# The second token group's seven taps summed by VectorE, and the first group's last sums taken in halves

## The chip, the cores and the metric

The kernel runs on one core of a Trainium2 chip. The metric is the device time of one execution in microseconds (us). Engines are named as in the profile: PE is TensorE, PEld its weight loads, DVE is VectorE, ACT is ScalarE, POOL is GpSimd and SP is SyncE, which here only issues DMAs.

## What is computed

A softmax-weighted causal convolution of 7 taps runs over the tokens, and a feed-forward layer follows it. Cut to what matters (B, S, D = 4, 4096, 192; H = 8 heads of 24 channels, K = 7 taps, d_ff = 2048):

```python
w = exp(weight_gen - max(weight_gen)); w = w / (sum(w) + 1e-9)      # per token and head, 7 taps
x_pad = concatenate([zeros(B, 6, D), x], axis=1)
conv[b, s, h, :] = sum over k of w[b, s, h, k] * x_pad[b, s + k, h, :]   # 24 channels a head
h = conv.reshape(16384, 192) @ w_in                                   # 192 -> 2048
g = where(h >= 1, h, where(h <= -1, 0, (h + 1)**2 / 4))
out = g @ w_out                                                       # 2048 -> 192
```

All values are fp32. The matmuls run in a reduced format (fp32r), so that each operand is split into a high part and a low part (what the high part leaves over), and products of high with high, low with high and high with low are added.

## The kernel before

**Layout.** The 16384 tokens lie in 32 lanes, and the 192 channels in 4 quads of 48, which gives 128 partitions. A group is 512 tokens (16 steps of each lane); there are 32 groups, worked in 16 pairs: `b` is 0 or 1 inside pair `pair`. Of a quad's 48 channels 32 are the main part and 16 the rest part. After the convolution a group is transposed by DVE, in blocks of 32 by 32, into `main_turn` and `rest_turn`; `xt_high` and `xt_low` are the high and low part of the turned main part, `xt_rest` holds both parts of the rest.

**The feed-forward loop.** For each group the 2048 hidden units are 16 tiles, n = 0 to 15. Tile n takes five matmuls into one of four PSUM banks (`slot`; line 815), by high and low weights `in_main_high`, `in_main_low`, `in_rest_high`, `in_rest_low`. Then ACT takes half_relu (L557), ACT squares it (L563), DVE clips it in place (L675, the gate), ACT copies the high part out (L568, gate_high) and DVE subtracts it (L681, gate_low). PE multiplies the gates of tile n - 4 with `out_parts`, the high and low part of w_out, in eight matmuls (L841), right after the hidden products of tile n (`LAG = 4`). PE may write tile n's slot only once the gate_low of tile n - 4 is done. Each engine works a queue written out by hand; what an engine does besides the tiles is put between two tiles by tables such as `HIGHS_AFTER`.

**The convolution.** In the loop POOL makes the convolution of the next group: seven products of `x_in` with a tap weight (L381) and six additions (L410, L418), all 128x768. The head of the program is different: group 0's convolution is made by DVE (taps 0 to 4) and POOL (taps 5 and 6), and PE adds the pieces with an identity matrix as stationary operand into PSUM (L851 main part, L854 rest part). Group 1 is convolved by POOL while PE works the 16 tiles of group 0.

**The weights.** High and low parts of w_in and w_out are made during the head and group 0, in pieces: ACT makes the high parts (`in_high`, `out_high`), and the low parts are subtractions. `in_low` pieces 0 to 3 (for tiles 0 to 7) are made by POOL in the head, pieces 4 to 7 by DVE after its gates of tiles 3, 4, 8 and 9 (L485). The four `out_low` pieces (L491) are POOL's. Piece c of `out_low` is needed by PE's outputs of tile 4c:

```python
wait(pe, gate_low_done, pair, 2 * NT, NT * b + n + 1)
if b == 0 and is_first(pair) and n % CT == 0:
    pe.wait_ge(out_low_done, n // CT + 1)
```

**Around the second group.** `rest_high` (ACT, L576) copies the rest part's high half, `rest_low` (POOL, L469) subtracts, DVE turns it (L712); the main part is turned (L702), copied (`main_high`, L581) and subtracted (`main_low`, L476).

## Time and profile before

| what | value |
| --- | --- |
| median of 3 runs | 1200.57 us (1200.52 to 1203.15) |
| the profiled execution's own time | 1203.05 us |
| span of the profiled execution | 1201.2 us |
| PE busy | 1191.7 us (99%) |
| DVE, ACT, POOL busy | 803.8 (67%), 899.9 (75%), 782.5 us (65%) |
| chain that ended last, by engine | PE 97%, DVE 1%, ACT 1% |

The span is the time from the first to the last instruction; the execution's own time has 1.85 us more, which lie outside it. The chain that ended last is followed back from the last instruction, at each step to what released it, so its shares say which engine sets the end. Of the three runs two lie at 1200.5 and one at 1203.15; the profiled one lies beside the third.

### The profile page before, as it was taken

The page shows a single profiled execution, that of the slowest core. Times are in us where ns is not written, and L with a number is a line of the kernel's source. Part 1 is how long each engine was busy: PE and PEld are TensorE (multiplying, and loading weights), DVE is VectorE, ACT ScalarE, POOL GpSimd, SP SyncE. Part 2 cuts the span into 40 slices and gives each one's busy share as a digit, 9 for nine tenths or more (in the row PEclk, how much of TensorE's full clock was granted, in tenths as well). Part 3 has the DMA queues.
Part 4 walks back from the last instruction along what each step waited for, and adds up shares of the span by engine and source line. Part 5 has one row for each costly group of instructions (what it writes and reads, how often), then busy time and mean ns, then how long its engine had stood idle before and what let it go on. Part 6 is the DMA issues. An engine that isn't in the chain of part 4 may idle for free.

```text
span 1201.2 us, 21341 instructions
## 1 busy us (share of the span) xinstructions
PE 1191.7 (99%) x6716; PEld 1071.9 (89%) x6716; DVE 803.8 (67%) x1331; ACT 899.9 (75%) x1775; POOL 782.5 (65%) x547
## 2 busy tenths in 40 slices
PE   8999999999999999999999999999999999999998
PEld 6889999898899999999989999899999998989888
DVE  6876666666666666666666666666666666666665
ACT  5877777777777777777777777777777777777775
POOL 7888577655677555776556776557765567765500
PEclk9999999999999999999999999999999999999999
DMA  8202122210222201222102222012221022220000
GB/s 170 40 13 57 21 44 44 44 40 4 44 44 44 44 22 21 44 44 44 35 8 44 44 44 44 22 21 44 44 44 35 8 44 44 44 44 22 1 36 14
DMA packets 172247, 45.33 MB, mean 38 GB/s; under 512 B 161220, under 2 KB 163652, under 8 KB 172228
## 3 DMA queue, kind: packets, MB, share of 16 engines
q1 hardware_dynamic: 167284, 44.29, 17.4%
q10 hardware_dynamic: 4944, 0.80, 0.5%
q8 instruction: 10, 0.16, 0.1%
q14 instruction: 9, 0.07, 0.0%
HBM read 24.62 MB, written 12.58 MB: 31 GB/s over the span
## 4 chain that ended last, share of the span: by engine, by line
PE 97%; DVE 1%; ACT 1%; POOL 0%; DMA 0%; issue 0%; ACTq 0%; DVEq 0%; POOLq 0%
PE slot L815 49%; PE acc L841 48%; DVE in_main_low L485 0%; DMA gen_in<-in_weight_gen 0%; PE slot L851 0%; POOL conv L528 0%; ACT gate_high L568 0%; ACT square L563 0%; POOL conv L381 0%; POOL out_cross L381 0%; DVE slot L675 0%; DVE gate_low L681 0%; ACT half_relu L557 0%; DVE out_sb L719 0%; PE acc L854 0%
## 5 line engine op out<-in xcount | busy, mean ns | idle before, releaser
L841 PE MATMUL acc<-out_parts,gate_high 128*128 128x384 f32 x2048 | 613.1, 355 | 0.0
L681 DVE TENSOR_TENSOR gate_low<-slot,gate_high 128x512 fp32r<-128x512 f32 x512 | 353.9, 691 | 384.1 <-ACT gate_high L568 384.1
L841 PE MATMUL acc<-out_parts,gate_low 128*128 128x192 f32 x2048 | 513.3, 251 | 0.0
L557 ACT ACTIVATE half_relu<-slot 128x512 f32<-128x512 f32 x512 | 308.1, 602 | 255.9 <-PE slot L815 248.8
L841 PEld LDWEIGHTS acc<-out_parts,gate_high 128*128 128x128 f32 x2048 | 384.8, 188 | 30.0 <-DVE out_sb L719 8.4
L841 PEld LDWEIGHTS acc<-out_parts,gate_low 128*128 128x128 f32 x2048 | 390.1, 190 | 18.4
L675 DVE SCALAR_TENSOR_TENSOR slot<-slot,square 128x512 f32<-128x512 f32 x512 | 353.2, 690 | 1.2 <-ACT square L563 1.2
L568 ACT ACTIVATE gate_high<-slot 128x512 fp32r<-128x512 f32 x512 | 304.0, 594 | 29.2 <-DVE slot L675 28.2
L563 ACT ACTIVATE square<-half_relu 128x512 f32<-128x512 f32 x512 | 324.4, 634 | 0.0
L381 POOL TENSOR_TENSOR tap<-x_in,tap_w 128x768 f32<-128x768 f32 x186 | 286.6, 1548 | 0.0
L410 POOL TENSOR_TENSOR conv<-conv,tap 128x768 f32<-128x768 f32 x124 | 229.5, 1851 | 0.0
L815 PE MATMUL slot<-xt_high,in_main_high 128*128 128x512 f32 x512 | 211.8, 414 | 3.2 <-DVE gate_low L681 3.1
L815 PE MATMUL slot<-xt_low,in_main_high 128*128 128x512 f32 x512 | 202.3, 395 | 0.1
L815 PE MATMUL slot<-xt_rest,in_rest_high 128*128 128x512 f32 x512 | 201.2, 393 | 0.0
L815 PE MATMUL slot<-xt_high,in_main_low 128*128 128x512 f32 x512 | 201.1, 393 | 0.0
L815 PE MATMUL slot<-xt_rest,in_rest_low 128*128 128x512 f32 x512 | 199.2, 389 | 0.0
L469 POOL TENSOR_TENSOR rest_parts<-conv,rest_parts 128x256 fp32r<-128x256 f32 x31 | 23.3, 751 | 174.6 <-ACT rest_parts L576 96.9
L815 PEld LDWEIGHTS slot<-xt_rest,in_rest_low 128*128 128x128 f32 x512 | 96.3, 188 | 23.2
L815 PEld LDWEIGHTS slot<-xt_rest,in_rest_high 128*128 128x128 f32 x512 | 96.0, 188 | 22.1
L815 PEld LDWEIGHTS slot<-xt_low,in_main_high 128*128 128x128 f32 x512 | 96.2, 188 | 21.6 <-DVE xt_low L476 0.5
L815 PEld LDWEIGHTS slot<-xt_high,in_main_high 128*128 128x128 f32 x512 | 96.3, 188 | 4.2 <-DVE gate_low L681 3.7
L815 PEld LDWEIGHTS slot<-xt_high,in_main_low 128*128 128x128 f32 x512 | 97.8, 191 | 0.1
(66 smaller groups left out, 532.1 us busy)
## 6 DMA issues: line engine op xcount, KB each, us to landing
x_in<-in_x SPq DMA_DIRECT2D x122, 132.0 KB, 3.0
out<-out_sb SPq DMA_DIRECT2D x31, 384.0 KB, 2.9
xt_rest<-rest_turn SPq DMA_DIRECT2D x30, 256.0 KB, 2.3
gen_in<-in_weight_gen SPq DMA_DIRECT2D x122, 28.0 KB, 2.2
out_raw<-in_moe_w_out SPq DMA_DIRECT2D x4, 384.0 KB, 5.1
in_main<-in_moe_w_in SPq DMA_DIRECT2D x8, 64.0 KB, 3.8
in_main<-in_moe_w_in SPq DMA_DIRECT2D x4, 128.0 KB, 4.4
in_rest<-in_moe_w_in SPq DMA_DIRECT2D x4, 128.0 KB, 4.4
```

What stands on the lines that cost most here:

```text
L381: return ops.tensor_tensor((dst if isinstance(dst, bass.AP) else dst[:]).rearrange("p t (h c) -> p t h c", h=HQ), x_in[b][:, k:k + STEP, : ...
L410: nc.gpsimd.tensor_tensor(to[:], conv[b][:], tap[k % 3][:], ALU.add).then_inc(conv_step, 1)
L469: return ops.tensor_tensor(rest_half(1), conv[b][:, :, MAIN:CH], rest_half(0).bitcast(F32), ALU.subtract)
L557: nc.scalar.activation(half_relu[n % 2][:], tile_slot(n)[:], ACT.Relu, scale=0.5, bias=0.5).then_inc(relu_done, 1)
L563: nc.scalar.activation(square[n % 2][:], half_relu[n % 2][:], ACT.Square).then_inc(square_done, 1)
L568: nc.scalar.activation(gate_high[GATE_AT[n]][:], tile_slot(n)[:], ACT.Copy).then_inc(gate_high_done, 1)
L675: nc.vector.scalar_tensor_tensor(h[:], h[:], 1.0, square[n % 2][:], ALU.max, ALU.min).then_inc(gate_done, 1)
L681: nc.vector.tensor_tensor(gate_low[GATE_AT[n]][:], tile_slot(n)[:], gate_high[GATE_AT[n]][:].bitcast(F32), ALU.subtract).then_inc(gate_low ...
L815: ins = nc.tensor.matmul(tile_slot(n)[:], w[:, units], xt[b][:], start=(j == 0), stop=(j == len(products) - 1))
L841: ins = nc.tensor.matmul(dst, stationary, moving, start=(n == 0 and j == 0), stop=(n == NT - 1 and j == 1))
```

## The change

Three things are changed. All lie in the head and in pair 0; the loop over the other pairs is the same code.

1. **Second group.** POOL makes only the seven products, into `second_taps`, a buffer with eight planes of 128x768. DVE adds them with six reductions over the tap axis (`second_sum`), whose innermost read step is one plane (768 elements). Three of them add planes 0 to 3 into plane 7 (the rest channels, then the main channels of steps 0 to 7, then of steps 8 to 15), after the gates of tiles 5, 6 and 7; three add planes 4 to 7 into `conv1`, after the gates of tiles 9, 10 and 11. Each makes 256 sums of 4 elements. `rest_high` comes after tile 10 on ACT, `rest_low` after it on POOL, the rest part is turned after tile 11, and its copy to `xt_rest` goes by DMA in place of ACT.
2. **Low parts.** `in_low` 4 to 7 move from DVE to POOL. `out_low` 2 moves from the middle of POOL's convolution to behind `rest_low`.
3. **First group.** Taps 5 and 6, whose sum POOL now adds in two halves (steps 0 to 7 and 8 to 15), are added by DVE and no longer by PE; the last sums, their transposes, `xt_high` and `xt_low` go in halves through two PSUM banks. PE's order in tiles 0 and 1 has the rest products ahead of the xt_low product. The second group's weight_gen is loaded after in_rest's second piece on ACT's DMA queue, and its exponent is taken after `xt_rest`.

```diff
-IN_LOWS_AFTER = {3: 4, 4: 5, 8: 6, 9: 7}
-HIGHS_AFTER = {1: ("out", 1), 2: ("in", 4), 3: ("in", 5), 5: ("out", 2), 7: ("in", 6), 8: ("in", 7),
+HIGHS_AFTER = {1: ("out", 1), 2: ("in", 4), 3: ("in", 5), 5: ("in", 6), 6: ("in", 7), 7: ("out", 2),
                9: ("out", 3)}
-OUT_LOWS_AFTER_TAP = {1: 1, 3: 2}
+EARLY_TAPS = 4
+SECOND_SUMS_AFTER = {5: (0, 0), 6: (0, 1), 7: (0, 2), 9: (1, 0), 10: (1, 1), 11: (1, 2)}
-FIRST_MAIN_AFTER, FIRST_REST_AFTER = (12, 9), (12, 12)
+FIRST_MAIN_AFTER, FIRST_REST_AFTER = (12, 9), (11, 12)
+SECOND_REST_HIGH_AFTER = 10
 SOFTMAX_AFTER = {2: ("max",), 7: ("sum", "inverse")}
-FIRST_SOFTMAX_AFTER = ({5: ("max",), 11: ("sum", "inverse")}, {2: ("max",), 10: ("sum", "inverse")})
-EXP_AFTER, FIRST_EXP_AFTER = 7, (11, 10)
-PAD_AFTER_TAP, SHIFT_AFTER_TAP = 2, 4
+FIRST_SOFTMAX_AFTER = ({8: ("max",), 13: ("sum", "inverse")}, {2: ("max",), 10: ("sum", "inverse")})
+EXP_AFTER, FIRST_EXP_AFTER = 7, (12, 10)
...
+        HALF = STEP // 2
+        first_main = [slot[i][:, 0:HALF * MAIN].rearrange("p (t c) -> p t c", c=MAIN) for i in (3, 1)]
+        first_turned = [t[:, 0:GT // 2].rearrange("p (i j r) -> p i j r", i=TOK, r=LANES) for t in (slot[2], acc[0])]
         first_rest = acc[TOK - 1][:, 0:STEP * REST].rearrange("p (t c) -> p t c", c=REST)
...
-                    if has_next(pair, b) and not (b == 0 and is_first(pair)):
+                    if has_next(pair, b):
...
+        def convolve_second(pool):
+            def taps(first, last):
+                for k in range(first, last):
+                    tap_product(nc.gpsimd, 1, k, second_taps[:, k]).then_inc(second_tap_made, 1)
+            pool.wait_ge(x_loaded[1], 16 * QUADS)
+            pool.wait_ge(taps_ready, 2)
+            taps(0, EARLY_TAPS)
+            out_low(pool, nc.gpsimd, 1).then_inc(out_low_done, 1)
+            in_low(pool, nc.gpsimd, 4).then_inc(in_low_done, 1)
+            in_low(pool, nc.gpsimd, 5).then_inc(in_low_done, 1)
+            pool.wait_ge(first_conv_done, 1)
+            nc.gpsimd.memset(x_in[0][:, 0:PAD, :], 0.0).then_inc(x_padded, 1)
+            taps(EARLY_TAPS, K)
+            in_low(pool, nc.gpsimd, 6).then_inc(in_low_done, 1)
+            in_low(pool, nc.gpsimd, 7).then_inc(in_low_done, 1)
...
                 if is_second(pair, b):
-                    out_low(pool, nc.gpsimd, W_CHUNKS - 1).then_inc(out_low_done, 1)
+                    out_low(pool, nc.gpsimd, 2).then_inc(out_low_done, 1)
+                    shift(pool, nc.gpsimd, *after(pair, b))
+                    out_low(pool, nc.gpsimd, 3).then_inc(out_low_done, 1)
...
-                nc.gpsimd.tensor_tensor(conv[1][:], conv[1][:], partial, ALU.add).then_inc(late_tap_step, 1)
+                for i in range(2):
+                    nc.gpsimd.tensor_tensor(steps_half(conv[1], i), steps_half(conv[1], i), steps_half(partial, i),
+                                            ALU.add).then_inc(late_tap_step, 1)
...
-                wait_conv(act, pair, b)
+                if is_second(pair, b):
+                    act.wait_ge(second_rest_summed, 1)
+                else:
+                    wait_conv(act, pair, b)
...
+            def first_main_high(i):
+                act.wait_ge(first_main_turned if i == 0 else main_turned, 1)
+                nc.scalar.activation(first_columns(xt_high[0], i), first_turned[i], ACT.Copy
+                                     ).then_inc(first_xt_high_done if i == 0 else xt_high_done, 1)
...
             for q in range(QUADS):
+                load_rest(act, 1, q)
+            for q in range(QUADS):
                 load_gen(act, 0, 1, q)
-            for q in range(QUADS):
-                load_rest(act, 1, q)
...
-            exponent(0, 1)
+            first_main_high(0)
             rest_high(0, 0)
-            main_high(0, 0)
+            first_main_high(1)
             out_high(0)
             act.wait_ge(rest_turned, 1)
             nc.scalar.activation(xt_rest[0][:], rest_turn[:], ACT.Copy).then_inc(first_xt_rest_done, 1)
+            exponent(0, 1)
...
-                        if n == main_after(pair, b) and has_next(pair, b):
+                        if n == rest_high_after(pair, b) and has_next(pair, b):
                             rest_high(*after(pair, b))
                         if n == main_after(pair, b) + 1 and has_next(pair, b):
                             main_high(*after(pair, b))
-                        if b == 0 and is_first(pair) and n == rest_after(pair, b) + 1:
-                            act.wait_ge(rest_turned, 2)
-                            nc.scalar.activation(xt_rest[1][:], rest_turn[:], ACT.Copy).then_inc(xt_rest_copied, 16)
...
+            def second_sum(late, piece):
+                steps, chans = ((slice(0, STEP), slice(MAIN, CH)), (slice(0, HALF), slice(0, MAIN)),
+                                (slice(HALF, STEP), slice(0, MAIN)))[piece]
+                taps = slice(EARLY_TAPS, K + 1) if late else slice(0, EARLY_TAPS)
+                to = conv[1][:] if late else second_taps[:, K]
+                dve.wait_ge(second_tap_made, K if late else EARLY_TAPS)
+                if late:
+                    dve.wait_ge(second_early_summed, piece + 1)
+                if late and piece == 2:
+                    dve.wait_ge(second_rest_summed, 1)
+                    dve.wait_ge(second_main_summed, 1)
+                done = (second_rest_summed, second_main_summed, conv_done)[piece] if late else second_early_summed
+                nc.vector.tensor_reduce(to[:, steps, chans],
+                                        second_taps[:, taps, steps, chans].rearrange("p k t c -> p t c k"),
+                                        AX.X, ALU.add).then_inc(done, 1)
...
+                for i in range(2):
+                    nc.vector.tensor_tensor(first_fourth[i], first_fourth[i], steps_half(tap[2], i), ALU.add
                                             ).then_inc(first_conv_step, 1)
-                tap_product(nc.vector, 0, 4, tap[2], first_taps_w).then_inc(first_conv_step, 1)
-                dve.wait_ge(first_conv_step, 4 + HQ)
-                dve.wait_ge(first_tap_summed, 1)
-                for h in range(HQ):
-                    nc.vector.tensor_tensor(head(conv[0], h), first_fourth[h], head(tap[2], h), ALU.add
+                    dve.wait_ge(first_conv_step, 7 + 2 * i)
+                    dve.wait_ge(late_tap_step, LATE + i + 1)
+                    nc.vector.tensor_tensor(steps_half(conv[0], i), first_fourth[i], steps_half(conv[1], i), ALU.add
                                             ).then_inc(first_conv_step, 1)
...
+            first_turn_main(0)
             softmax(0, 1, "max")
-            shift(dve, nc.vector, 0, 1)
-            turn_main(0, 0)
+            first_turn_main(1)
             dve.wait_ge(rest_high_done, 1)
             nc.vector.tensor_tensor(rest_half(1), first_rest, rest_half(0).bitcast(F32), ALU.subtract
                                     ).then_inc(first_rest_low_done, 1)
             turn_rest(0, 0)
-            dve.wait_ge(xt_high_done, 1)
-            main_low(nc.vector, 0, 0).then_inc(first_xt_low_done, 1)
+            shift(dve, nc.vector, 0, 1)
+            for i in range(2):
+                dve.wait_ge(first_xt_high_done if i == 0 else xt_high_done, 1)
+                nc.vector.tensor_tensor(first_columns(xt_low[0], i), first_turned[i],
+                                        first_columns(xt_high[0], i).bitcast(F32), ALU.subtract
+                                        ).then_inc(first_xt_low_done, 1)
...
-            sum_tap(conv[0], first_conv_step, 1, first=True)
-            sum_tap(tap[0], first_conv_step, 2)
-            sum_tap(tap[1], first_conv_step, 3)
-            sum_tap(conv[1], late_tap_step, LATE + 1)
-            sum_tap(conv[0], first_conv_step, 4 + 2 * HQ, last=True)
+            sum_tap(conv[0], 1, first=True)
+            sum_tap(tap[0], 2)
+            sum_tap(tap[1], 3)
+            pe.wait_ge(first_conv_step, 8)
+            sum_main(conv[0], 0, last=True)
+            pe.wait_ge(first_conv_step, 10)
+            sum_rest(conv[0], last=True)
+            sum_main(conv[0], 1, last=True)
             warm(WARM_PRODUCTS[1])
             for n in range(2):
-                hidden_products(0, 0, n, 0, 2)
+                hidden_products(0, 0, n, (0, 1), opens=True, closes=False)
             for n in range(2):
-                hidden_products(0, 0, n, 2, 3)
+                hidden_products(0, 0, n, (3, 4, 2), opens=False, closes=True)
```

On POOL, from the end of the head to the end of its work for the second group, the instructions stood so before (L381 products, L410 and L418 additions, L491 out_low pieces 1, 2 and 3, L469 `rest_low`):

```order
L410 TENSOR_TENSOR conv<-conv,tap 128x768 [waits conv_step]
L491 TENSOR_TENSOR out_parts<-out_raw,out_parts 128x4x192 [waits out_high_done]
L381 TENSOR_TENSOR tap<-x_in,tap_w 128x768
L410 TENSOR_TENSOR conv<-conv,tap 128x768 [waits conv_step]
L452 TENSOR_TENSOR gen_shift<-gen_in,gen_max 128x224 [waits exp_done,max_done]
L381 TENSOR_TENSOR tap<-x_in,tap_w 128x768
L410 TENSOR_TENSOR tap<-conv,tap 128x768 [waits conv_step]
L418 TENSOR_TENSOR conv<-tap 128x768 [waits conv_step]
L469 TENSOR_TENSOR rest_parts<-conv,rest_parts 128x256 [waits rest_high_done]
L491 TENSOR_TENSOR out_parts<-out_raw,out_parts 128x4x192 [waits out_high_done]
L476 TENSOR_TENSOR xt_low<-main_turn,xt_high 128x512 [waits xt_high_done]
```

Here the first L491 is `out_low` 2, which waits for nothing but its high part. In the changed kernel (L394 products, L510 in_low pieces 4 to 7, L516 out_low pieces, L495 `rest_low`):

```order
L394 TENSOR_TENSOR second_taps<-x_in,tap_w 128x768 x3
L516 TENSOR_TENSOR out_parts<-out_raw,out_parts 128x4x192 [waits out_high_done]
L510 TENSOR_TENSOR in_main_low<-in_main,in_main_high 128x512 [waits in_high_done]
L510 TENSOR_TENSOR in_rest_low<-in_rest,in_rest_high 128x512 [waits in_high_done]
L439 MEMSET x_in 128x288 [waits first_conv_done]
L394 TENSOR_TENSOR second_taps<-x_in,tap_w 128x768 x3
L510 TENSOR_TENSOR in_main_low<-in_main,in_main_high 128x512 [waits in_high_done]
L510 TENSOR_TENSOR in_rest_low<-in_rest,in_rest_high 128x512 [waits in_high_done]
L495 TENSOR_TENSOR rest_parts<-conv,rest_parts 128x256 [waits rest_high_done]
L516 TENSOR_TENSOR out_parts<-out_raw,out_parts 128x4x192 [waits out_high_done]
L475 TENSOR_TENSOR gen_shift<-gen_in,gen_max 128x224 [waits exp_done,max_done]
L516 TENSOR_TENSOR out_parts<-out_raw,out_parts 128x4x192 [waits out_high_done]
```

`out_low` 2, the L516 behind L495, now stands behind an instruction that waits for `rest_high_done`.

On DVE, between the gates (L675) of tiles 3 to 5, before:

```order
L675 SCALAR_TENSOR_TENSOR slot<-slot,square 128x512 [waits square_done]
L485 TENSOR_TENSOR in_main_low<-in_main,in_main_high 128x512 [waits in_high_done]
L681 TENSOR_TENSOR gate_low<-slot,gate_high 128x512 [waits gate_high_done]
L675 SCALAR_TENSOR_TENSOR slot<-slot,square 128x512 [waits square_done]
L485 TENSOR_TENSOR in_rest_low<-in_rest,in_rest_high 128x512 [waits in_high_done]
L681 TENSOR_TENSOR gate_low<-slot,gate_high 128x512 [waits gate_high_done]
```

and in the changed kernel from the gate (L713) of tile 5 to that of tile 8 (L719 is gate_low, L756 the new reductions):

```order
L713 SCALAR_TENSOR_TENSOR slot<-slot,square 128x512 [waits square_done]
L756 TENSOR_REDUCE second_taps<-second_taps 128x16x16 [waits second_tap_made]
L719 TENSOR_TENSOR gate_low<-slot,gate_high 128x512 [waits gate_high_done]
L713 SCALAR_TENSOR_TENSOR slot<-slot,square 128x512 [waits square_done]
L756 TENSOR_REDUCE second_taps<-second_taps 128x8x32 [waits second_tap_made]
L719 TENSOR_TENSOR gate_low<-slot,gate_high 128x512 [waits gate_high_done]
L713 SCALAR_TENSOR_TENSOR slot<-slot,square 128x512 [waits square_done]
L756 TENSOR_REDUCE second_taps<-second_taps 128x8x32 [waits second_tap_made]
L719 TENSOR_TENSOR gate_low<-slot,gate_high 128x512 [waits gate_high_done]
L713 SCALAR_TENSOR_TENSOR slot<-slot,square 128x512 [waits square_done]
L699 TENSOR_REDUCE gen_max<-gen_in 128x32 [waits shift_done,gen_loaded0]
```

The two L485 between the gates are gone, and three reductions have come in two tiles later.

## Rows read from the trace of the kernel before

**Rows 1.** The page: busy time by engine, and the chain by engine.

```profile
PE 1191.7 (99%) x6716; PEld 1071.9 (89%) x6716; DVE 803.8 (67%) x1331; ACT 899.9 (75%) x1775; POOL 782.5 (65%) x547
PE 97%; DVE 1%; ACT 1%; POOL 0%; DMA 0%; issue 0%; ACTq 0%; DVEq 0%; POOLq 0%
```

**Rows 2.** Waits of PE: who for whom, us in total, times, longest.

```profile
PE slot L815 <- DVE gate_low L681: 3.1, 2, 2.6
```

**Rows 3.** PE's timeline: start, us busy, and in brackets idle before.

```profile
21.86 0.50 PE L815 MATMUL slot<-xt_high,in_main_high 128*128 128x512 f32 x1 [0.46 <-DVE gate_low L681]
...
31.61 0.50 PE L815 MATMUL slot<-xt_high,in_main_high 128*128 128x512 f32 x1 [2.61 <-DVE gate_low L681]
...
53.86 0.41 PE L815 MATMUL slot<-xt_high,in_main_high 128*128 128x512 f32 x1
...
56.15 0.41 PE L815 MATMUL slot<-xt_high,in_main_high 128*128 128x512 f32 x1
```

**Rows 4.** DVE's timeline, group 0: the gates of tiles 3, 7 and 8.

```profile
25.96 0.69 DVE L675 SCALAR_TENSOR_TENSOR slot<-slot,square 128x512 f32<-128x512 f32 x1
26.56 4.39 DVE L485 TENSOR_TENSOR in_main_low<-in_main,in_main_high 128x512 fp32r<-128x512 f32 x1
...
37.62 0.69 DVE L675 SCALAR_TENSOR_TENSOR slot<-slot,square 128x512 f32<-128x512 f32 x1
39.02 0.69 DVE L681 TENSOR_TENSOR gate_low<-slot,gate_high 128x512 fp32r<-128x512 f32 x1 [0.72 <-ACT gate_high L568]
39.63 0.69 DVE L675 SCALAR_TENSOR_TENSOR slot<-slot,square 128x512 f32<-128x512 f32 x1
```

**Rows 5.** POOL's timeline, group 0.

```profile
28.60 1.79 POOL L410 TENSOR_TENSOR conv<-conv,tap 128x768 f32<-128x768 f32 x1
30.35 0.33 POOL L413 MEMSET x_in<- 128x288 f32 x1
...
34.55 1.85 POOL L491 TENSOR_TENSOR out_parts<-out_raw,out_parts 128x768 fp32r<-128x768 f32 x1
...
49.29 0.74 POOL L469 TENSOR_TENSOR rest_parts<-conv,rest_parts 128x256 fp32r<-128x256 f32 x1 [3.01 <-ACT rest_parts L576]
```

**Rows 6.** Windows: busy PE, PEld, DVE, ACT, POOL; granted clock; DMA share, GB/s.

```profile
32.00:36.00 4.00, 4.00 (x15) 3.63 (x14) 3.36 (x7) 3.81 (x7) 4.00 (x3) 0.57 0.47 82
```

**Rows 7.** The head's timeline: DVE, PE and ACT.

```profile
11.38 1.02 DVE L739 TENSOR_TENSOR conv<-acc,tap 128x384 f32<-128x384 f32 x2
...
14.76 0.73 DVE L702 STREAM_TRANSPOSE slot<-slot 128x512 f32<-128x512 f32 x1 [1.63 <-PE slot L851]
...
16.18 0.50 PE L815 MATMUL slot<-xt_high,in_main_high 128*128 128x512 f32 x1
...
16.84 0.63 ACT L622 ACTIVATE xt_rest<-rest_turn 128x512 fp32r<-128x512 f32 x1
...
17.43 0.50 PE L815 MATMUL slot<-xt_low,in_main_high 128*128 128x512 f32 x1
```

**Rows 8.** Groups of instructions by form: busy us, mean ns, idle before.

```profile
L665 DVE TENSOR_REDUCE gen_sum<-gen_exp 128x32 f32<-128x256 f32 x31 | 12.7, 410 | 0.5 <-ACT gen_exp L552 0.5
...
L702 DVE STREAM_TRANSPOSE main_turn<-conv 128x512 f32<-128x512 f32 x31 | 34.5, 1111 | 0.0
```

**Rows 9.** ACT's timeline, group 0.

```profile
39.91 0.61 ACT L557 ACTIVATE half_relu<-slot 128x512 f32<-128x512 f32 x1
40.39 0.62 ACT L568 ACTIVATE gate_high<-slot 128x512 fp32r<-128x512 f32 x1
40.86 0.66 ACT L563 ACTIVATE square<-half_relu 128x512 f32<-128x512 f32 x1
41.38 0.87 ACT L612 ACTIVATE out_parts<-out_raw 128x768 fp32r<-128x768 f32 x1
42.12 0.63 ACT L557 ACTIVATE half_relu<-slot 128x512 f32<-128x512 f32 x1
...
48.78 0.43 ACT L576 ACTIVATE rest_parts<-conv 128x256 fp32r<-128x256 f32 x1
```

119 lines of the change are left out of this document (66 added, 53 removed).

## Prediction

> **What bounds the kernel now.** I read the page first: PE is busy 99% of the span and makes 97% of the chain that ended last [rows 1]. So only two things can move the end: what PE does, which the change leaves alone, and when PE stands still or runs slow. The waits of PE come next: the longest is 2.6 us, for a gate_low [rows 2], and PE's timeline places it ahead of tile 7 of the first group, 31.61 us, 2.61 us idle [rows 3]. Then the other engines there. DVE's timeline: an `in_main_low` that began at 26.56 took 4.39 us, and the gate_low that PE wanted stood behind it [rows 4]. POOL's timeline: an addition that reads SBUF ended at 30.39, a memset began at 30.35, and DVE's subtraction ended at 30.95, 0.6 us later [rows 5]. So DVE waited for POOL with a two-input operation from SBUF, and not for its data. After the stall the windows show a granted clock of 0.57 over 32 to 36 us [rows 6], between the levels of 1.2 and 2.4 GHz: 4.00 x (1 - 0.57) = 1.72 us of PE's work is lost.
>
> From tile 4's start at 21.86 to the second group's first tile at 53.86 are 12 tiles [rows 3]. A tile at full pace is 2.29 us (53.86 to 56.15), so they would take 27.44. They took 32.00: 4.56 us are lost, of which 2.61 is the stall, 1.72 the clock, and 0.23 the restart.
>
> **The change, part by part. In_low on POOL.** DVE loses its four two-input SBUF subtractions, and with them the 4.39. All that is left of two-input work in this stretch reads PSUM with one input. This gives back the 2.61 of the stall, and the 1.95 behind it if no new stall follows. On POOL, two 128x512 subtractions take the place of two 128x768 additions ahead of the memset, so both end before the 30.35 of [rows 5], and tile 8, which needs them, starts at 30.7 (below). Then come three products and two subtractions, none longer than the 1.85 of an `out_low`: at most 9.3, to 39.6, for tile 12 at 39.86. I cost the move at nothing.
>
> **The head.** In before, PE added POOL's partial sum and then DVE's last one, and the main part was turned at 14.76 after 1.63 us of waiting; the two additions on DVE took 1.02 [rows 7]. Now DVE makes four such halves (2 x 1.02, from 11.38 to 13.43), and PE has 0.44 us of rest and a half main part left behind them, so the second main half is ready at about 14.55, 0.2 earlier. Its transpose and its copy are half as long (about 0.45 for the 0.73), so the first product comes near 15.6 for 16.18. But tile 0 also needs the rest part: high half, subtraction, transpose and the 0.63 copy, which ended at 17.47 and now ends about 0.35 earlier, at 17.1. The rest products then start there, where before PE went on at 17.43 with `xt_low` [rows 7]. Halves, warm-up and loads taken together: a gain of 0.3 us, with bounds of 0 and 0.6 (the first product's own gain).
>
> **The reductions.** Each reads 4 x 256 = 1024 elements with a step of one plane. The trace has no such read. Lower bound: the reduction of 256 elements took 0.410 us [rows 8] and a gate of 512 took 0.69 [rows 4], 1.09 ns for each element more; 768 more make 1.25 us. Upper bound: the transposes that write with a step took 1.111 us [rows 8] where the first, with runs, took 0.73 [rows 7], 0.74 ns more an element; on 1024 elements that is 0.76, so 2.01 us. I take 1.25, since it is the same operation.
>
> A rule of the Trainium skill speaks for the upper bound. Its page "Vector Engine (DVE) Microarchitecture Reference", section 5.2, measures about 1.73 ns a column where one source hops by 4 KiB at every element, against 1.05 for contiguous reads; by it a reduction would take about 1.85 us (an estimate from the page). The same section tells of a one-source operation alternating between two regions at full rate, which is why it does not settle the matter. No row here shows either.
>
> DVE's pace in this stretch is set by a ring: gate, gate_high, gate. The gates of tiles 7 and 8 are 2.01 us apart [rows 4], with 0.72 idle. A reduction of 1.25 fills the idle time: gate_low 0.61, gate 0.60, reduction 1.18 from start to start make 2.39, 0.38 more than without, and 0.10 above PE's 2.29. Gate 3 came at 25.96, 4.1 us after PE began tile 4, and PE needs its gate_low only for tile 7, 6.9 us after tile 4's start. So PE does not wait for gates here, but DVE does not catch up either.
>
> **The new wait.** `out_low` 2, which PE needs for the outputs of tile 8 (right after the hidden products of tile 12), stood at 34.55 [rows 5], 10 us early. Now it is behind `rest_low`, which waits for `rest_high`, which stands on ACT after tile 10. In steps, with the head's 0.3 off:
> - PE: tile 4 at 21.56; tile 12 at 21.56 + 8 x 2.287 = 39.86; it wants outputs 8 behind its five products, a little over half a tile, at 39.86 + 1.17 = 41.03.
> - DVE: gate 3 at 25.96 - 0.3 = 25.66 [rows 4]; gates 4 and 5 at +2.0 each, 29.66; gates 6, 7, 8 at +2.39 each, 36.83.
> - ACT: gate_high 8 at 36.83 + 0.74 = 37.57; then by the start-to-start times of [rows 9]: square 9 +0.48, `out_high` 3 +0.52, half_relu 10 +0.74, gate_high 9 +0.48, square 10 +0.47, `rest_high` +0.52: 40.78. It takes 0.43 [rows 9]: 41.21.
> - POOL: `rest_low` at 41.26, `out_low` 2 from 41.96 (0.70 on, a little under its 0.74) for 1.85 [rows 5]: 43.81. PE goes on at 43.86.
>
> PE stands 43.86 - 41.03 = 2.83 us. That is a little more than the stall that goes, so the granted clock should fall behind it as it did before: 1.95 us again with the restart.
>
> **Sum.** Stall of before -2.61, its clock and restart -1.95, head -0.3, new wait +2.83, its clock and restart +1.95: -0.08 us. Against the profiled execution's 1203.05 us this is 1203.0. That execution stands 0.2% above the median of 1200.57, beside the slowest of the three. Perhaps in the other two DVE got its turn one boundary of POOL's earlier (at 28.60 for 30.35, 1.75 us less, and with a wait of PE under 1 us perhaps no clock loss, 3.5 in all at most): they differ by 2.6. In the changed kernel this chance is gone, as no DVE operation waits for POOL's port. So I expect 1203.0 and not the same distance below the median. After tile 12 the second group's inputs are on time: the transposes of tiles 11 and 12 and `main_low` end over 1 us before PE's first product that reads them, since PE itself is late by 2.8.
>
> **Rivals.**
> - *The wait comes, the clock stays up* (0.14). The gap is a little shorter or the engine's activity around it is other than at 29 to 31 us. The sum loses 1.7: 1201.3.
> - *The strided reads are slow* (0.26, the other side). Each reduction takes 2.01; a tile with one lasts 0.61 + 0.60 + 1.94 = 3.15 on DVE. Gate 8 comes 3 x 0.76 = 2.28 later, and `rest_high` waits for the fourth reduction, about 0.6 more: PE loses 2.9 more, part of it ahead of tiles 10 and 11 on gate_low: 1203.0 + 2.9 = 1205.9. It decides from about 1.6 us a reduction. For it speak the transposes; against it, that reductions of before ran at one element a cycle. The page's rule above is this case; its 1.85 would give about 1205.3, by the same steps.
> - *No new wait* (0.12). ACT and DVE are further ahead at tile 10 than I reckon, and `out_low` 2 comes by 41.03. Then both stalls are gone: 1203.0 - 2.83 - 1.95 = 1198.2. Against it speaks gate 3's distance of 4.1 us from tile 4's start, which is of the same work in both kernels.
> - *The distance of the two kinds of runs of before has nothing to do with the stall* (0.1). Then the changed kernel's usual run lies 0.1 below the median: 1200.5.
> - *My forecast*: 0.38, its own range 1202.0 to 1204.0, by the head's bounds and 0.7 us of error in the chain.
>
> **How the numbers follow.** The range is to leave out 2 in 10: about half of the slow-reduction case above, and the better half of the no-wait case below: 1199.0 to 1206.0. About what a measurement can tell from no change here is 0.3%, 3.6 us: faster is below 1197.0, which needs no new wait and a head gain over 1 us (0.05); slower is above 1204.2, the slow-reduction case and the edge of mine (0.29); the rest is the same (0.66).
>
> **What would show it.** No L510 on DVE and no wait of PE ahead of tile 7; a wait of PE of 2.8 us near 41 us at L905, released by POOL's L516; the granted clock down for some 3 us behind it; L756 at 1.2 us; the first hidden product near 15.6 and half_relu of tile 0 near 18.1. The prediction is wrong if L756 takes over 1.6 us, if L516's third run ends before 41 us, or if PE waits for the second group's `xt_high`.

## The result, and the profile after

| kernel | median | runs | range | granted clock |
| --- | --- | --- | --- | --- |
| before | 1200.83 us | 7 | 1200.52 to 1203.23 | 0.998 in the profiled one |
| changed | 1206.17 us | 7 | 1205.54 to 1207.22 | 0.996 to 0.999 |

The changed kernel is slower: ratio 1.0039, with a 95% interval of 1.0027 to 1.0050. Its profiled execution took 1207.13 us with a span of 1205.3, 4.1 us more than before's 1201.2. The seven runs of each kernel lie in two groups, those of before at 1200.5 to 1200.8 and at 1203.1 to 1203.2, those of the changed kernel at 1205.5 to 1206.2 and at 1207.1 to 1207.2, and both profiles are of the upper group.

The page of the changed kernel, to be held against [rows 1]: busy time by engine, then the chain that ended last.

```profile
PE 1191.7 (99%) x6720; PEld 1073.1 (89%) x6720; DVE 807.8 (67%) x1337; ACT 898.9 (75%) x1775; POOL 774.9 (64%) x546
...
PE 96%; POOL 2%; issue 1%; DMA 1%; DVE 0%; ACTq 0%; ACT 0%; DVEq 0%; POOLq 0%
```

PE is busy for the same 1191.7 us, so in sum the 4.1 us are time in which PE stands still. What is new in the chain is POOL with 2%, and issue and DMA with 1% each. The waits of PE, against [rows 2]:

```profile
PE acc L905 <- POOL out_parts L516: 3.9, 1, 3.9
PE slot L879 <- DVE gate_low L719: 1.6, 3, 0.6
```

The 2.6 us for a gate_low are gone, and 3.9 us for `out_low` have come, with three shorter waits for gate_low. PE's timeline places them; against [rows 3]:

```profile
16.72 0.47 PE L879 MATMUL slot<-xt_high,in_main_high 128*128 128x512 f32 x1 [0.68 <-issue]
...
22.39 0.51 PE L879 MATMUL slot<-xt_high,in_main_high 128*128 128x512 f32 x1 [0.48 <-DVE gate_low L719]
...
36.93 0.50 PE L879 MATMUL slot<-xt_high,in_main_high 128*128 128x512 f32 x1 [0.57 <-DVE gate_low L719]
...
40.06 0.50 PE L879 MATMUL slot<-xt_high,in_main_high 128*128 128x512 f32 x1 [0.59 <-DVE gate_low L719]
...
42.44 0.41 PE L879 MATMUL slot<-xt_high,in_main_high 128*128 128x512 f32 x1
...
47.66 0.66 PE L905 MATMUL acc<-out_parts,gate_high 128*128 128x384 f32 x1 [3.88 <-POOL out_parts L516]
...
58.08 0.41 PE L879 MATMUL slot<-xt_high,in_main_high 128*128 128x512 f32 x1
```

These are tile 0's first product, tile 4, tiles 10, 11 and 12, the outputs of tile 8, and the second group's first tile. Tile 4 starts 0.53 us later than before (22.39 for 21.86). From there to the second group are 12 tiles of 2.287 us, 27.44 in all; they took 35.69, so 8.25 are lost where before lost 4.56. The two differences, 0.53 and 3.69, make 4.22, which is the span's 4.1.

DVE's timeline where the reductions stand (L756), and later the fourth of them:

```profile
30.46 0.69 DVE L713 SCALAR_TENSOR_TENSOR slot<-slot,square 128x512 f32<-128x512 f32 x1
31.06 2.06 DVE L756 TENSOR_REDUCE second_taps<-second_taps 128x256 f32<-128x1024 f32 x1
33.01 0.70 DVE L719 TENSOR_TENSOR gate_low<-slot,gate_high 128x512 fp32r<-128x512 f32 x1
33.60 0.71 DVE L713 SCALAR_TENSOR_TENSOR slot<-slot,square 128x512 f32<-128x512 f32 x1
...
42.49 1.97 DVE L756 TENSOR_REDUCE conv<-second_taps 128x256 f32<-128x1024 f32 x1
```

A reduction takes 2.06 us, and the gates before and after it (L713) are 3.14 us apart, where PE's tile takes 2.29. DVE falls behind by 0.85 us a tile. POOL's work does not make the reductions slow: the fourth takes 1.97 us while POOL stands idle (next rows). POOL's timeline behind `in_low`:

```profile
35.95 1.28 POOL L510 TENSOR_TENSOR in_rest_low<-in_rest,in_rest_high 128x512 fp32r<-128x512 f32 x1
45.00 0.73 POOL L495 TENSOR_TENSOR rest_parts<-conv,rest_parts 128x256 fp32r<-128x256 f32 x1 [7.78 <-ACT rest_parts L611]
45.69 1.82 POOL L516 TENSOR_TENSOR out_parts<-out_raw,out_parts 128x768 fp32r<-128x768 f32 x1
```

POOL stands idle for 7.78 us with `out_low` 2 (the L516 at 45.69) behind an instruction that waits for the rest part, and the rest part waits for the fourth reduction. The window from the end of PE's long wait on has, after its length, busy PE, PEld, DVE, ACT and POOL, the granted clock, and DMA share and GB/s:

```profile
46.00:52.00 6.00, 4.34 (x13) 3.96 (x14) 6.00 (x6) 2.69 (x6) 3.84 (x3) 0.50 0.01 3
```

The clock is at the lower of its two levels, 1.2 GHz, for the whole stretch. In the head, DVE's timeline against [rows 7]:

```profile
7.22 0.95 DVE L394 TENSOR_TENSOR conv<-x_in,acc 128x768 f32<-128x768 f32 x1 [0.43 <-DMA x_in<-in_x]
...
13.88 0.46 DVE L734 STREAM_TRANSPOSE slot<-slot 128x256 f32<-128x256 f32 x1
15.45 0.39 DVE L699 TENSOR_REDUCE acc<-gen_in 128x32 f32<-128x224 f32 x1 [1.11 <-DMA gen_in<-in_weight_gen]
15.75 0.45 DVE L734 STREAM_TRANSPOSE acc<-slot 128x256 f32<-128x256 f32 x1
```

The first row is DVE's first tap product. Between the two half transposes of group 0 stands the maximum of the second group's weight_gen (L699). It waited 1.11 us for its DMA, with the second half's transpose behind it.

### The profile page after: what moved, and what is told of

It is laid out like the page before. It is cut to its first block, busy times and chain, and to the rows that moved or that the text cites. A ratio compares the mean times of both kernels' runs of the same rounds, so it can differ in the third digit from the quotient of the medians.

```text
span 1205.3 us, 21360 instructions
## 1 busy us (share of the span) xinstructions
PE 1191.7 (99%) x6720; PEld 1073.1 (89%) x6720; DVE 807.8 (67%) x1337; ACT 898.9 (75%) x1775; POOL 774.9 (64%) x546
## 4 chain that ended last, share of the span: by engine, by line
PE 96%; POOL 2%; issue 1%; DMA 1%; DVE 0%; ACTq 0%; ACT 0%; DVEq 0%; POOLq 0%
PE slot L879 49%; PE acc L905 47%; POOL second_taps L394 1%; DMA gen_in<-in_weight_gen 1%; POOL out_parts L516 0%; POOL in_main_low L510 0%; POOL in_rest_low L510 0%; ACTq L297 0%; ACTq L270 0%; DVE out_sb L774 0%; DVE gen_shift L475 0%; POOL rest_parts L495 0%; DVE xt_low L820 0%; DVE gen_sum L703 0%; DVE tap_w L484 0%
## 5 line engine op out<-in xcount | busy, mean ns | idle before, releaser
L905 PE MATMUL acc<-out_parts,gate_high 128*128 128x384 f32 x2048 | 613.6, 356 | 3.9 <-POOL out_parts L516 3.9
L719 DVE TENSOR_TENSOR gate_low<-slot,gate_high 128x512 fp32r<-128x512 f32 x512 | 353.6, 691 | 384.8 <-ACT gate_high L600 384.8
L905 PE MATMUL acc<-out_parts,gate_low 128*128 128x192 f32 x2048 | 513.5, 251 | 0.0
L905 PEld LDWEIGHTS acc<-out_parts,gate_high 128*128 128x128 f32 x2048 | 385.1, 188 | 34.1 <-DVE out_sb L774 8.4
L905 PEld LDWEIGHTS acc<-out_parts,gate_low 128*128 128x128 f32 x2048 | 390.4, 191 | 18.4
L713 DVE SCALAR_TENSOR_TENSOR slot<-slot,square 128x512 f32<-128x512 f32 x512 | 353.0, 689 | 0.8 <-ACT square L595 0.8
L394 POOL TENSOR_TENSOR tap<-x_in,tap_w 128x768 f32<-128x768 f32 x180 | 277.5, 1549 | 0.0
L422 POOL TENSOR_TENSOR conv<-conv,tap 128x768 f32<-128x768 f32 x120 | 222.3, 1853 | 0.0
L495 POOL TENSOR_TENSOR rest_parts<-conv,rest_parts 128x256 fp32r<-128x256 f32 x31 | 23.1, 745 | 180.8 <-ACT rest_parts L611 97.2
```

The costliest lines, as they stand in the source:

```text
L394: return ops.tensor_tensor((dst if isinstance(dst, bass.AP) else dst[:]).rearrange("p t (h c) -> p t h c", h=HQ), x_in[b][:, k:k + STEP, : ...
L422: nc.gpsimd.tensor_tensor(to[:], conv[b][:], tap[k % 3][:], ALU.add).then_inc(conv_step, 1)
L495: return ops.tensor_tensor(rest_half(1), conv[b][:, :, MAIN:CH], rest_half(0).bitcast(F32), ALU.subtract)
L713: nc.vector.scalar_tensor_tensor(h[:], h[:], 1.0, square[n % 2][:], ALU.max, ALU.min).then_inc(gate_done, 1)
L719: nc.vector.tensor_tensor(gate_low[GATE_AT[n]][:], tile_slot(n)[:], gate_high[GATE_AT[n]][:].bitcast(F32), ALU.subtract).then_inc(gate_low ...
L905: ins = nc.tensor.matmul(dst, stationary, moving, start=(n == 0 and j == 0), stop=(n == NT - 1 and j == 1))
```

## The experiments

The first four ran on one chip, the last four on another, each beside runs of the kernel before (medians 1201.02 of 23 and 1200.71 of 24). All ratios are to before. The changed kernel was not measured again beside them, and its median of 1206.17 is the uppermost of the lower group of its runs, so differences to it below are good to about half a us.

### `out_low` 2 ahead of `rest_low`

The changed kernel with `out_low` 2 put back ahead of the wait:

```diff
             in_low(pool, nc.gpsimd, 7).then_inc(in_low_done, 1)
+            out_low(pool, nc.gpsimd, 2).then_inc(out_low_done, 1)
...
                 if is_second(pair, b):
-                    out_low(pool, nc.gpsimd, 2).then_inc(out_low_done, 1)
                     shift(pool, nc.gpsimd, *after(pair, b))
```

> The changed kernel with out_low piece 2 back ahead of rest_low on GpSimd, right after in_low 7. Theory 1 (the wait of 3.9 us sits on that piece's place): the wait at the outputs of tile 8 and the clock loss behind it go; but the second group's xt_high and xt_low stay as late as they are (ACT 53.8 us, GpSimd 54.5 to 55.8 us), so PE stands again ahead of tile 13 to 15 on gate_low and at the second group's first tile, which begins near 55 us for 58.1: 2 to 3 us faster than the changed kernel, about 1203.5. Rival (the wait is only the visible end of DVE's backlog): PE stands just as long in other places and the time does not move by more than 1 us, 1205.5 to 1206.5. Second rival (the whole loss goes): 3.9 plus the clock's 2.4, about 1200.

1204.66 us (7 runs, 1204.53 to 1205.13), ratio 1.0027, interval 1.0015 to 1.0038. The wait at L905 is gone and the clock is 1.00 from 40 to 54 us, but PE's timeline now has this:

```profile
47.78 0.50 PE L879 MATMUL slot<-xt_high,in_main_high 128*128 128x512 f32 x1 [0.61 <-DVE gate_low L719]
51.81 0.50 PE L879 MATMUL slot<-xt_high,in_main_high 128*128 128x512 f32 x1 [1.50 <-DVE gate_low L719]
```

PE waits for gate_low six times, 4.0 us in all. So the wait for `out_low` covered a second one: DVE, late by six reductions of 2 us, does not keep up either. Taking the 3.88 us wait away alone brings 1.5 us. The place of the waits is as expected (tiles 13 to 15), the time is not: the gain lies between the 2 to 3 us of the expectation and the rival's 1.

### The reductions made contiguous

The changed kernel with `second_taps` laid out with the taps innermost, so that a reduction reads four neighbouring elements for each sum, and POOL's products write with a step of eight elements:

```diff
-        second_taps = sb("second_taps", [P, K + 1, STEP, CH])
+        second_taps = sb("second_taps", [P, STEP, CH, K + 1])
...
-                    tap_product(nc.gpsimd, 1, k, second_taps[:, k]).then_inc(second_tap_made, 1)
+                    tap_product(nc.gpsimd, 1, k, second_taps[:, :, :, k]).then_inc(second_tap_made, 1)
...
-                                        second_taps[:, taps, steps, chans].rearrange("p k t c -> p t c k"),
+                                        second_taps[:, steps, chans, taps],
```

> The changed kernel with the tap axis innermost in second_taps, so that DVE's reductions read 4 neighbouring elements and GpSimd's products write with a step of 32 bytes. Theory 1 (the read's step costs 0.8 us a reduction): reductions 1.2 to 1.3 us for 2.0, the gate_low waits ahead of tiles 10 and 11 go, the wait at out_low 2 shrinks from 3.9 to about 2.8, total about 3 us faster: 1203. Rival (a sum of 4 in 1024 elements takes 2 us however it is read): reductions stay at 2.0 us and the time at 1206. Open: what the stepped writes cost GpSimd; if its products take 2.3 for 1.5 us, the four late planes come 5 us later, at 42 us, and the gain shrinks.

1202.66 us (11 runs, 1200.72 to 1204.47), ratio 1.0009, interval 1.0000 to 1.0018. The groups by form (busy us, mean ns, idle before):

```profile
L394 POOL TENSOR_TENSOR second_taps<-x_in,tap_w 128x768 f32<-128x768 f32 x7 | 11.4, 1781 | 0.0
L756 DVE TENSOR_REDUCE second_taps<-second_taps 128x256 f32<-128x1024 f32 x3 | 3.6, 1210 | 0.0
```

The same groups in the changed kernel:

```profile
L394 POOL TENSOR_TENSOR second_taps<-x_in,tap_w 128x768 f32<-128x768 f32 x7 | 10.6, 1543 | 0.3 <-DVE tap_w L484 0.3
L756 DVE TENSOR_REDUCE second_taps<-second_taps 128x256 f32<-128x1024 f32 x3 | 6.2, 2065 | 0.0
```

The reduction falls from 2.065 to 1.210 us, and POOL's product pays 0.24 us, which nothing waits for. The waits for gate_low past tile 4 are gone; the one for `out_low` is shorter:

```profile
43.60 0.41 PE L905 MATMUL acc<-out_parts,gate_high 128*128 128x384 f32 x1 [2.44 <-POOL out_parts L516]
...
53.23 0.41 PE L879 MATMUL slot<-xt_high,in_main_high 128*128 128x512 f32 x1
```

The second row is the second group's first tile. Tile 4 started at 21.44, so the 12 tiles took 31.79 us and 4.35 are lost, where the changed kernel lost 8.25. In the medians the strided layout costs 3.5 us, though these runs spread over 3.75.

### The load of weight_gen first

The changed kernel with the second group's weight_gen ahead of in_rest's second piece on ACT's DMA queue, as before had it:

```diff
             for q in range(QUADS):
-                load_rest(act, 1, q)
+                load_gen(act, 0, 1, q)
             for q in range(QUADS):
-                load_gen(act, 0, 1, q)
+                load_rest(act, 1, q)
```

> The changed kernel with the second group's weight_gen loaded ahead of in_rest's second piece on ACT's DMA queue, as before the change. Theory 1 (the late landing at 15.42 us holds the second half's transpose behind the max): max at about 13.9, second transpose at about 14.9 for 15.75, first hidden product near 15.7 for 16.72; the head is 0.5 to 0.9 us shorter, and so is the time: 1205.3 to 1205.7 if the stalls behind keep their length. Rival (in_rest's second piece comes too late then, or the stalls swallow it): no change within 0.3 us, since the wait at out_low 2 hangs on DVE's chain which starts earlier too, or since in_rest is on the path.

1205.55 us (5 runs, 1205.34 to 1206.84), ratio 1.0039, interval 1.0025 to 1.0053. DVE's timeline:

```profile
6.81 0.95 DVE L394 TENSOR_TENSOR conv<-x_in,acc 128x768 f32<-128x768 f32 x1 [0.26 <-DMA x_in<-in_x]
...
13.82 0.35 DVE L699 TENSOR_REDUCE acc<-gen_in 128x32 f32<-128x224 f32 x1
14.76 0.47 DVE L734 STREAM_TRANSPOSE acc<-slot 128x256 f32<-128x256 f32 x1 [0.59 <-PE slot L914]
```

The maximum no longer waits, and the second transpose waits for PE, as it should. The first product starts at 15.74 for 16.72 and tile 4 at 21.48 for 22.39. Not all of these 0.9 us are the load's: this profile's head also began earlier, with DVE's first product at 6.81 for 7.22, once `x_in` had landed. The profile of the first experiment tells the two apart, since its first product starts at 7.22 as in the changed kernel and only the maximum comes earlier:

```profile
7.22 0.95 DVE L394 TENSOR_TENSOR conv<-x_in,acc 128x768 f32<-128x768 f32 x1
...
14.63 0.40 DVE L699 TENSOR_REDUCE acc<-gen_in 128x32 f32<-128x224 f32 x1 [0.31 <-DMA gen_in<-in_weight_gen]
15.18 0.47 DVE L734 STREAM_TRANSPOSE acc<-slot 128x256 f32<-128x256 f32 x1 [0.15 <-PE slot L914]
```

Its tile 4 starts at 21.82, so the late load costs 0.57 us in the changed kernel's profile (22.39), and the other 0.34 are the later start of the head. In the medians the edit brings 0.6 us, less than the spread of the changed kernel's runs, whose lower ones lie at 1205.5 to 1205.6 as well. The load isn't always this late: with the changed kernel's order of loads the maximum started at 15.45 in the profile of after, at 14.63 in that of the first experiment and at 14.37 in that of the second, where tile 4 started at 21.44.

### All three together

The edits of the three experiments above in one kernel:

```diff
-        second_taps = sb("second_taps", [P, K + 1, STEP, CH])
+        second_taps = sb("second_taps", [P, STEP, CH, K + 1])
...
             in_low(pool, nc.gpsimd, 7).then_inc(in_low_done, 1)
+            out_low(pool, nc.gpsimd, 2).then_inc(out_low_done, 1)
...
             for q in range(QUADS):
-                load_rest(act, 1, q)
+                load_gen(act, 0, 1, q)
```

> All three edits together. Theory 1 (each loss is its own): no wait at out_low 2, reductions 1.25 us, the head shorter: no wait of PE over 0.6 us after 20 us, second group's first tile near 50 to 51 us: 1198 to 1199.5, below both kernels. Rival (the second group's main part is late anyway, since DVE is about 3 us behind at tile 12): its first tile near 53, about 1201.

1199.71 us (11 runs, 1199.41 to 1199.98), ratio 0.9984, interval 0.9975 to 0.9993: 6.5 us less than the changed kernel, and less than before. PE's timeline at tile 4, at the second group's first tile and behind it:

```profile
21.47 0.50 PE L879 MATMUL slot<-xt_high,in_main_high 128*128 128x512 f32 x1 [0.47 <-DVE gate_low L719]
...
49.01 0.41 PE L879 MATMUL slot<-xt_high,in_main_high 128*128 128x512 f32 x1
...
50.16 0.50 PE L879 MATMUL slot<-xt_low,in_main_high 128*128 128x512 f32 x1 [0.50 <-POOL xt_low L503]
```

From 21.47 to 49.01 are 27.54 us for 12 tiles: nothing but 0.1 is lost. The one wait left in this part is 0.5 us for the second group's `xt_low`. The median is 0.2 above the 1198 to 1199.5 that was expected.

### Two of them, without the load

All three, with the loads back in the changed kernel's order, to see what the load is worth where the rest is out of the way:

```diff
             for q in range(QUADS):
-                load_gen(act, 0, 1, q)
+                load_rest(act, 1, q)
             for q in range(QUADS):
-                load_rest(act, 1, q)
+                load_gen(act, 0, 1, q)
```

> The changed kernel with two of the three edits: out_low 2 ahead of rest_low, and the tap axis innermost; the second group's weight_gen stays behind in_rest's second piece. Theory 1: without a stall of PE that follows, the head's late landing costs in full what it costs in the head, 0 to 0.9 us by where weight_gen lands (14.4 to 15.4 us in the runs so far against the 13.8 at which DVE is ready): 1199.7 to 1200.6, with a wider spread than with all three edits. Rival (the landing is hidden in any case): 1199.7 as with all three.

1199.66 us (11 runs, 1199.34 to 1200.79), ratio 0.9985, interval 0.9976 to 0.9994. The median is that of all three, but the runs spread over 1.45 us where those of all three spread over 0.57. Six of its runs lie at or below 1199.7, as those of all three do, and five at 1200.1 to 1200.8. So the late load may cost nothing in half of the runs and up to 1.1 us in the others, but that is argued from the spread alone: the only profiled run is one of 1199.66 us, where the maximum waited 0.35 us. The two edits without it explain the whole 6.5 us between the medians; alone they bring 1.5 and 3.5, 5.0 in sum. Together they bring more, since either alone leaves PE a wait that the other takes away: 4.0 us for gate_low in the first experiment, 2.44 us for `out_low` in the second.

### The second group's main part turned a tile earlier

All three, with `FIRST_MAIN_AFTER` at 11 in place of 12, against the last wait:

```diff
-FIRST_MAIN_AFTER, FIRST_REST_AFTER = (12, 9), (11, 12)
+FIRST_MAIN_AFTER, FIRST_REST_AFTER = (11, 9), (11, 12)
```

> All three edits, and the second group's main part is turned one tile earlier, behind tile 11's gate, so that xt_high and xt_low come earlier; the rest part's turn comes behind it, 1 us later. With all three edits PE waited 0.50 us for xt_low at tile 16 (released at 50.11). If that wait is worth its length: 0.5 us faster, 1199.2. Rival: both turns in one tile hold DVE 1 us, gate_low of tile 11 comes at 46.8 where PE wants it at 46.7, or the copy of the rest part by DMA lands after 49.7: the same or slower by up to 0.5 us.

1200.56 us (10 runs, 1200.26 to 1200.93), ratio 0.9990, interval 0.9981 to 0.9999; 0.9 above all three and above the two without the load, which were on the same chip; the rival had 0.5 at most. The wait for `xt_low` is gone, but DVE makes both transposes in one tile (45.63 to 47.5), and the gate_low behind them comes at 47.50. PE's longest wait for `out_sb` has also grown, from 0.5 to 1.2 us. The profile is of the slowest run (1200.93), whose head is 0.67 us longer than that of all three (tile 4 at 22.14 for 21.47); from tile 4 on PE's timeline has this:

```profile
48.22 0.50 PE L879 MATMUL slot<-xt_high,in_main_high 128*128 128x512 f32 x1 [0.64 <-DVE gate_low L719]
```

### Before, with only the subtractions moved

The kernel before, with `in_low` 4 to 7 on POOL and nothing else changed:

```diff
-IN_LOWS_AFTER = {3: 4, 4: 5, 8: 6, 9: 7}
+IN_LOWS_AFTER_TAP = {1: (4, 5), 3: (6, 7)}
...
+                if is_second(pair, b) and k in IN_LOWS_AFTER_TAP:
+                    for half in IN_LOWS_AFTER_TAP[k]:
+                        in_low(pool, nc.gpsimd, half).then_inc(in_low_done, 1)
```

> The kernel before with its four in_low pieces 4 to 7 moved from DVE to GpSimd (behind its taps 1 and 3) and nothing else. Theory 1 (DVE's two-input subtractions wait for GpSimd, and GpSimd has no room for more): DVE has no instruction over 1.2 us, the wait of 2.6 us ahead of tile 7 and the half clock behind it go; but the second group's convolution ends 4 to 5 us later, near 49 to 51 us, so PE waits 2 to 5 us at the second group's first tile: 1200 to 1204. Rival (the 4.39 us on DVE came from its data or its turn, not from GpSimd): the wait of PE ahead of tile 7 stays or moves to a near tile, and the time is above 1205. It also tells the two kinds of runs apart: if they (2.5 us apart) come from when DVE gets its turn, they are gone here.

1205.28 us (8 runs, 1203.99 to 1205.60), ratio 1.0032, interval 1.0021 to 1.0043. PE doesn't wait ahead of tile 7, and no operation of DVE in this stretch takes over 1.2 us, as expected. But POOL's convolution, now with four subtractions in it, ends at 50.05, and DVE waits for it with a gate_low of PE's behind it. First POOL's last addition and DVE's transpose, then PE's first product of the second group:

```profile
48.21 1.84 POOL L421 TENSOR_TENSOR conv<-tap 128x768 f32<-128x768 f32 x1
...
50.08 1.11 DVE L705 STREAM_TRANSPOSE main_turn<-conv 128x512 f32<-128x512 f32 x1 [2.53 <-POOL conv L421]
...
53.06 0.79 PE L816 MATMUL slot<-xt_high,in_main_high 128*128 128x512 f32 x1 [3.43 <-DVE gate_low L684]
```

The wait is within the expected 2 to 5 us, and the time is above the expected 1200 to 1204: the granted clock is 0.50 from 52 until after 58 us, and the expectation had no price for that. So POOL has no room for the subtractions unless something else leaves it, which in the changed kernel the additions do. And the two sorts of runs of before, 2.5 us apart, are not seen: seven of the eight lie within 0.6 us, one 1.0 lower.

### Before once more

The kernel before without a change of its work, to profile a run of its other sort:

```diff
-LAG = 4
+LAG = 2 + 2
```

> The kernel before once more, to catch a profile of its other kind of run (about 1200.6). Theory 1: in that one in_main_low on DVE ends at a boundary of GpSimd before 30.35, at 28.6 or 27.1, it takes about 2.6 or 1.2 us for 4.39, and PE waits 0 to 0.9 us ahead of tile 7. Rival (the two kinds come from the head's DMA or from the granted clock alone): the same 4.39 us and the same wait, and the difference is in the head or in the windows' clock.

1200.5 us in its one run, span 1198.7. DVE's and POOL's timelines, for [rows 4] and [rows 5]:

```profile
26.55 1.13 DVE L485 TENSOR_TENSOR in_main_low<-in_main,in_main_high 128x512 fp32r<-128x512 f32 x1
...
27.09 1.99 POOL L381 TENSOR_TENSOR tap<-x_in,tap_w 128x768 f32<-128x768 f32 x1
29.04 2.31 POOL L410 TENSOR_TENSOR conv<-conv,tap 128x768 f32<-128x768 f32 x1
```

Here DVE got its turn when POOL's `out_low` ended at 27.09, and POOL's product paid with 1.99 us for its 1.54. The same subtraction, begun at the same time, takes 1.13 us in place of 4.39. PE's timeline has tile 7 at 28.83 with no wait, the granted clock is 1.00 throughout, and tile 16 comes at 49.80:

```profile
28.83 0.41 PE L815 MATMUL slot<-xt_high,in_main_high 128*128 128x512 f32 x1
...
49.80 0.50 PE L815 MATMUL slot<-xt_high,in_main_high 128*128 128x512 f32 x1 [0.21 <-DVE gate_low L681]
...
51.13 0.50 PE L815 MATMUL slot<-xt_low,in_main_high 128*128 128x512 f32 x1 [0.60 <-POOL xt_low L476]
```

Tile 16 comes 4.06 us earlier than in [rows 3], and the span is 2.5 us shorter. The rest goes to waits that the profile of [rows 3] does not have: 0.21 and 0.60 us here and 0.7 later for `out_sb`, with the restarts.

## Where the prediction held and where it failed, step by step

The forecast was 1203.0, with a range of 1199.0 to 1206.0, and the measured median is 1206.17, at the upper edge. Against the median of before the forecast was 2.4 us more and the measurement is 5.3 more. The mechanism of the new wait is as forecast. The rival of the slow strided reads, 1205.9, is what happened, and by the prediction's own sign, a reduction over 1.6 us, the forecast is wrong.

**The step that failed is the reduction's price.** The forecast had bounds of 1.25 and 2.01 us from rows of before and took 1.25, "since it is the same operation". Measured are 2.07 and 1.96 in the mean of the first and the last three: the upper bound. It was the better row, since what costs is how the elements lie and not which operation reads them: contiguous, the same reduction takes 1.21, close to the 1.25. That it fits so closely is in part luck, as its rows are transposes that write with a step, and the reductions read with one. The Trainium skill's page "Vector Engine (DVE) Microarchitecture Reference", section 5.2, gives more time for one source that hops far at every element; the estimate of 1.85 us from it was nearer than 1.25, and the case agrees with it in kind, at 1.96 to 2.07.

**What hangs on it.** The forecast's steps on the path to `out_low` 2 hold once the right price is in. With 1.25 they gave 43.81 for its end, with 2.01 the rival added 2.88; tile 4 started 0.83 later than forecast (22.39 for 21.56). That makes 47.5, and the row shows 45.69 + 1.82. The second experiment is the other half of the proof: with 1.21 a reduction it has a wait of 2.44 for 2.83, and 4.35 us lost from tile 4 to the second group where the forecast's wait, clock and restart make 4.78. Its median of 1202.66 fits as well, but its runs spread from 1200.7 to 1204.5, and that says less.

**Where the 4.3 us between forecast and profile lie.** The forecast's sum was -0.08; PE's timeline gives 4.22. The terms:

| term | forecast | measured | difference |
| --- | --- | --- | --- |
| head, to tile 4 | -0.3 | +0.53 | 0.83 |
| tiles 4 to 12 beyond full pace | 0 | 1.75 (1.16 of waits for gate_low, the rest restarts) | 1.75 |
| wait for `out_low` 2 | 2.83 | 3.88 | 1.05 |
| clock and restart behind it | 1.95 | 2.62 | 0.67 |
| before's loss that goes | -4.56 | -4.56 | 0 |

The 1.75 is 42.44 less 22.39 less 8 x 2.287, and the 2.62 is what the 8.25 leave. The two middle terms that hang on the reductions make 2.80, close to the rival's 2.9; the head and the clock come on top, and no rival had them. The forecast said that PE would not wait for gates; that is right at 1.21 and wrong at 2.06, as the second experiment shows. `in_low` on POOL cost nothing, as forecast: its pieces end at 29.93 and 37.23, and tiles 8 and 12 start at 31.62 and 42.44.

**The wait came, as forecast.** The mechanism, an `out_low` behind an instruction that waits for the rest part, is right, in its place and its releaser. What the forecast did not say is that it stood in front of a second one. The first experiment shows that: without it DVE's backlog comes out at tiles 13 to 15 and takes back more than half of the gain.

**The head.** The forecast's 0.3 us holds where the inputs land in time: in the profile of all three edits DVE's first product starts at 6.87, as in before, and tile 4 at 21.47, 0.39 before [rows 3]. Two things are missing in the forecast. One is the load moved behind in_rest on ACT's queue, which was named among the changes and not costed: 0.57 us in the profiled run. The other is that the changed head has lost slack. In the six profiles with the change and a maximum by 14.63, tile 4 starts 14.60 to 14.67 us after DVE's first product, so the 0.35 us by which that product was later than in before (7.22 for 6.87) are paid in full; in the two profiles of before it starts at 6.87 and 7.16, and tile 4 at 21.86 and 21.85. The three make the table's term: -0.39 + 0.57 + 0.35 = 0.53.

**The stall of before was the wrong thing to subtract.** The forecast found it in the profiled execution, whose time lies beside the upper sort of before's runs, and supposed that the other sort had its turn earlier. The profile of such a run bears that out, and goes further: DVE gets in already at 27.09, there is no wait ahead of tile 7 and no clock loss, and the run is 2.55 us shorter. A little over half of before's runs are of this sort (27 of the 47 on the two chips of the experiments). So the change takes away a stall that the median run, it seems, doesn't have. That the stall comes from these subtractions is shown by their removal from DVE, after which it is gone. The Trainium skill's page "SBUF — State Buffer", section "Who interferes with whom", says that a DVE instruction with two SBUF inputs contends with a GpSimd instruction that reads SBUF, and that a reduction never does. This case agrees: 1.13 or 4.39 us for one subtraction, and 1.21 for each contiguous reduction, beside POOL's products and without them.

**Open.** After its wait of 3.88 us, which ended at 47.66, the changed kernel ran at 1.2 GHz until after 52 us. Windows of the changed kernel, with the granted clock third from last:

```profile
45.50:46.00 0.50, 0.00 (x0) 0.00 (x0) 0.50 (x2) 0.30 (x1) 0.50 (x2) 0.86 0.00 0
...
50.00:52.00 2.00, 2.00 (x6) 1.58 (x6) 2.00 (x3) 0.14 (x1) 0.00 (x0) 0.50 0.00 0
```

With the load first, after a wait of 3.86 us that ended at 46.72, the clock was back soon after 50 us:

```profile
46.50:47.00 0.50, 0.28 (x1) 0.31 (x2) 0.50 (x2) 0.00 (x0) 0.50 (x2) 0.84 0.00 0
...
50.00:52.00 2.00, 2.00 (x12) 1.81 (x12) 2.00 (x4) 0.77 (x2) 0.00 (x0) 0.94 0.03 11
```

In the one the clock fell before 46 us, while PE still waited, in the other just after PE had gone on. From tile 4 to the second group's first tile the one took 35.69 us and the other 34.87. The 0.8 us between these may be what parts the changed kernel's own two sorts of runs, 1205.5 to 1206.2 at a clock of 0.999 and 1207.1 to 1207.2 at 0.996 or 0.997. What decides between them no run here shows. That DVE's turn is what parts the two sorts of before is argued too: from one profile of each, and from eight runs without the subtractions on DVE that do not lie 2.5 us apart. How often it gets its turn at which boundary, and why, stays open.

## What to carry to other kernels

Price an operation by the nearest row with the same way of stepping through memory, not by the nearest row of the same name; and where one of two bounds turns the sign of the sum, lay the data out so that the cheap one holds, if a producer with idle time (here POOL) can pay. Before a wait is removed or a stall is credited, look at what the same run would wait for next, and whether the median run has the stall at all: the profiled execution may be of another sort. Never put something that the critical engine needs soon behind a wait for something that it needs late.

## What the runs showed of the hardware

- A reduction over four planes 3072 bytes apart reads 1024 elements in 1.96 to 2.07 us; with the four elements side by side it takes 1.21.
- A GpSimd product of 128x768 that writes fp32 with a step of 32 bytes takes 1.78 us, contiguously 1.54 (1.60 in the first experiment): the writer loses 0.24 where the reader gains 0.85.
- A DVE subtraction that waits for GpSimd can miss its turn at two boundaries between GpSimd's instructions (27.10 and 28.60 us) and get it at the third (30.35), or get it at the first (27.09): 4.39 or 1.13 us for an instruction that starts within 0.01 us of the same time. The two profiled executions differ by 2.55 us of 1200.
- Behind a PE wait of 1.50 us the granted clock stayed at 1.00; with waits of 2.44, 2.61, 3.43, 3.86 and 3.88 it was at its lower level for a time, and not always for the same time: until after 52 us behind the wait that ended at 47.66, until soon after 50 behind the one that ended at 46.72.
